# First tile's outputs from the second weight as loaded, in float32 products; the weight's split moved one step on

## The reference

```
attention:  a = softmax(causal(q k^T / 8));  local = a @ v            32 heads (4 x 8), 576 rows, 64 columns
            mem = (phi(q) @ M_prev) / (phi(q) . z_prev)
            x = g * mem + (1 - g) * local                             -> x: 2304 x 512
stage 1:    h = x @ w_in                                              512 -> 1024
            solu = h * softmax(h);  ln = (solu - mean) / sqrt(var + 1e-6) * g_ln
            y = ln @ w_out                                            1024 -> 512
stage 2:    out = (sigmoid(y @ w_gate) * (y @ w_val)) @ w_out2        512 -> 1536 -> 512
```

## Time and profile before

| | |
|---|---|
| median of 3 runs | 836.41 us (835.51 to 836.73) |
| the profiled execution | 835.18 us |
| its span | 833.4 us |
| PE busy | 814.7 us (98%) |
| DVE busy | 604.4 us (73%) |
| ACT busy | 465.4 us (56%) |
| POOL busy | 20.7 us (2%) |
| granted TensorE clock, mean | 0.998 |

### The profile page before, as it was taken

How to read it: one execution, slowest core, us unless ns; L and a number is a source line. 1 busy time by engine, 2 the same in 40 slices (tenths; PEclk the granted TensorE clock), 3 DMA queues, 4 the chain that set the end, 5 groups by cost and what they waited for, 6 DMA issues and landing times.

```text
span 833.4 us, 15447 instructions
## 1 busy us (share of the span) xinstructions
PE 814.7 (98%) x5718; PEld 688.1 (83%) x5718; DVE 604.4 (73%) x1460; ACT 465.4 (56%) x965; POOL 20.7 (2%) x35
## 2 busy tenths in 40 slices
PE   7997999999999999999999999999999999999998
PEld 4555777777777778888899999999999999999997
DVE  7988888777777775686656777787677678666654
ACT  7988666666666653463535454564444465444443
POOL 1000000000000000111000000000000000000000
PEclk9999999999999999999999999999999999999999
DMA  7362011111111000100323011122111113111002
GB/s 217 93 194 61 17 52 53 53 52 54 53 50 39 26 17 15 52 1 1 101 77 126 26 51 52 52 61 98 45 52 50 52 42 111 51 52 51 26 1 77
DMA packets 67370, 48.99 MB, mean 59 GB/s; under 512 B 9568, under 2 KB 57952, under 8 KB 67296
## 3 DMA queue, kind: packets, MB, share of 16 engines
q1 hardware_dynamic: 67152, 47.74, 19.2%
q10 hardware_dynamic: 144, 0.26, 0.1%
HBM read 43.27 MB, written 4.72 MB: 58 GB/s over the span
## 4 chain that ended last, share of the span: by engine, by line
PE 89%; DVE 5%; SPq 2%; issue 2%; ACT 1%; DMA 1%; DVEq 0%; ACTq 0%
PE tt_bk L1622 10%; PE tt_bk L1624 10%; PE tt_bk L1623 10%; PE m_bk L1467 9%; PE s_bk L1491 7%; PE o_bk L1491 5%; PE tt_bk L1390 4%; PE s_bk L1674 3%; PE s_bk L1675 3%; PE s_bk L1673 3%; PE o_bk L1398 3%; PE s_bk L1326 3%; PE m_bk L1674 2%; PE m_bk L1675 2%; PE s_bk L1467 2%; PE m_bk L1673 2%
## 5 line engine op out<-in xcount | busy, mean ns | idle before, releaser
L1622 PE MATMUL tt_bk<-xc_hi,wc_hi 128*128 128x384 f32 x476 | 160.0, 336 | 0.0
L1624 PE MATMUL tt_bk<-xc_hi,wc_lo 128*128 128x384 f32 x476 | 160.0, 336 | 0.0
L1623 PE MATMUL tt_bk<-xc_lo,wc_hi 128*128 128x384 f32 x476 | 159.8, 336 | 0.0
L598 ACT ACTIVATE p_nat<-p_nat,negmax 128x512 f32<-128x512 f32 (+2 forms) x144 | 83.0, 578 | 46.6 <-DVE negmax L931 46.6
L1166 DVE TENSOR_TENSOR wc_lo<-wc_raw,wc_hi 128x768 fp32r<-128x768 f32 x72 | 78.3, 1088 | 31.9 <-ACT wc_hi L663 31.9
L1622 PEld LDWEIGHTS tt_bk<-xc_hi,wc_hi 128*128 128x128 f32 x476 | 89.4, 188 | 6.4 <-DVE c_u L1182 0.3
L1623 PEld LDWEIGHTS tt_bk<-xc_lo,wc_hi 128*128 128x128 f32 x476 | 89.4, 188 | 6.1
L1624 PEld LDWEIGHTS tt_bk<-xc_hi,wc_lo 128*128 128x128 f32 x476 | 89.4, 188 | 0.0
L663 ACT CAST wc_hi<-wc_raw 128x768 fp32r<-128x768 f32 x72 | 64.5, 946 | 1.3 <-DVE wc_raw L1160 1.3
L605 ACT COPY pT<-tt_bk 128x512 f32<-128x512 f32 (+1 forms) x87 | 46.0, 554 | 29.2 <-PE tt_bk L1390 27.8
L1390 PE MATMUL tt_bk<-ident,p_nat 128*128 128x128 f32 x400 | 56.0, 277 | 2.6 <-DVE pT L975 1.4
(11 more groups left out here) (219 smaller groups left out, 1773.7 us busy)
## 6 DMA issues: line engine op xcount, KB each, us to landing
wc_raw<-in_moe_w_val SPq DMA_DIRECT2D x36, 256.0 KB, 3.0
wc_raw<-in_moe_w_gate SPq DMA_DIRECT2D x36, 256.0 KB, 3.4
qkT<-in_q SPq DMA_DIRECT2D x15, 288.0 KB, 2.9
v_raw<-in_v SPq DMA_DIRECT2D x16, 256.0 KB, 2.7
qkT<-in_k SPq DMA_DIRECT2D x15, 256.0 KB, 3.2
out<-o_sb SPq DMA_DIRECT2D x15, 256.0 KB, 2.2
w_raw<-in_moe_w_out SPq DMA_DIRECT2D x12, 256.0 KB, 4.7
turned<-in_k SPq DMA_DIRECT2D x32, 72.0 KB, 2.6
```

The source lines that it names most:

```text
L598: nc.scalar.activation(p_tile(g, tile), p_tile(g, tile), ACT.Exp, bias=negmax[:, n:n + 1], scale=-1.0, accum_out=den[:, n:n + 1]).then_inc ...
L1622: mm(o, hi[:, k, c, :], xc_hi[:, j, c, :], start=start and c == 0, stop=False, skip_group_check=True)
L1623: mm(o, hi[:, k, c, :], xc_lo[:, j, c, :], start=False, stop=False, skip_group_check=True)
L1624: last = mm(o, lo[:, k, c, :], xc_hi[:, j, c, :], start=False, stop=c == 1, skip_group_check=True)
```

## The change

Tile 0's outputs are no longer made of three split products. VectorE's new `first_ln` multiplies the turned rows by `g_ln` into `u_even`, and TensorE's new `first_out` multiplies that with the loaded blocks of `w_out` in float32: 8 products instead of 24. ScalarE's and VectorE's split of tile 0's rows goes. The split of `w_out`, first needed by tile 1 now, moves: on both engines blocks 0 and 1 to step 5, 2 to 4 to step 6, 5 to 7 to step 7. In step 5 fill 4 of pair 4 is copied by ScalarE instead of VectorE, ahead of `moe_exp(0)`; VectorE's copy of fill 3 moves ahead of `moe_max(0)`. In TensorE's step 6 the order of `moe_hidden`, turns and outputs is another.

```diff
     def act_fills(g):
-        return [0, 2, 5, 6] if g == HP else [0, 2, 4, 5, 6]
+        return [0, 2, 4, 5, 6]
...
-        W2_HI_MID, W2_HI_X, W2_HI_TILE, W2_HI_END = {4: (0, 1)}, {5: (2, 3, 4)}, {5: (5, 6)}, {5: (7,)}
-        W2_LO_PHI, W2_LO_TILE = {4: (0, 1)}, {5: (2, 3, 4), 6: (5, 6, 7)}
+        W2_HI_X, W2_HI_TILE, W2_HI_END = {6: (2, 3, 4), 7: (5, 6, 7)}, {5: (0,)}, {5: (1,)}
+        W2_LO_MAX, W2_LO_ROWS, W2_LO_VAR = {5: (0,), 6: (2,), 7: (5, 6)}, {6: (3,), 7: (7,)}, {5: (1,), 6: (4,)}
...
 ScalarE, step(g, t)
-                if t == 1:
-                    moe_ln(t - 1)
...
                 keep_pt(g - 1, 2)
+                if t == 0:
+                    keep_pt(g - 1, 4)
                 if t == 1:
                     feature_relu(g + 1)
                 for f in W2_HI_TILE.get(g, ()):
                     split_w2(f)
                 moe_exp(t)
-                if 4 in act_fills(g - 1):
+                if t:
                     keep_pt(g - 1, 4)
...
 VectorE
+            def first_ln():
+                dve.wait_ge(g_in, 16)
+                for n in range(2):
+                    dve.wait_ge(lnt_ready, n + 1)
+                    c = slice(512 * n, 512 * n + 512)
+                    nc.vector.tensor_tensor(u_even[:, c].rearrange("p (f k) -> p f k", f=4),
+                                            t_bk[n][:, :].rearrange("p (f k) -> p f k", f=4),
+                                            g_col[:, 4 * n:4 * n + 4].unsqueeze(2).broadcast_to([P, 4, P]),
+                                            ALU.mult).then_inc(ln_lo_ok, 1)
...
-                if t:
+                if t == 1:
+                    first_ln()
+                elif t:
                     moe_ln_low(t - 1)
...
                 if t == 0:
-                    split_w2(W2_LO_TILE[g][0])
                     unit_max(g, 6)
-                    split_w2(W2_LO_TILE[g][1])
                 keep_pt(g - 1, 1)
-                if t < 2:
-                    split_w2(W2_LO_TILE[g][2 if t == 0 else 0])
+                if t == 0:
+                    keep_pt(g - 1, 3)
+                for f in W2_LO_MAX.get(g, ()):
+                    split_w2(f)
                 moe_max(t)
-                keep_pt(g - 1, 3)
-                if t == 0:
-                    keep_pt(g - 1, 4)
-                if t == 1:
-                    split_w2(W2_LO_TILE[g][1])
-                    split_w2(W2_LO_TILE[g][2])
+                if t:
+                    keep_pt(g - 1, 3)
+                for f in W2_LO_ROWS.get(g, ()):
+                    split_w2(f)
                 moe_rows(t)
                 moe_stats(t)
                 if t == 0:
                     unit_max(g + 1, 0)
                     unit_max(g + 1, 1)
+                for f in W2_LO_VAR.get(g, ()):
+                    split_w2(f)
                 moe_var(t)
...
 TensorE
+            def first_out(f0, f1):
+                if f0 == 0:
+                    pe.wait_ge(ln_lo_ok, 2)
+                    pe.wait_ge(w2_in, 16 * FB)
+                for f in range(f0, f1):
+                    last = mm(y_bank(False), u_even[:, f * P:(f + 1) * P], w2_stage(f)[:, 0, :], start=f == 0,
+                              stop=f == FB - 1)
+                if f1 == FB:
+                    last.then_inc(y_ready, 1)
...
+                if t == 1:
+                    moe_hidden(t, 12, 24)
+                    turn_p(g - 1, 0)
+                    turn_p(g - 1, 1)
+                    pe.wait_ge(max_ok, NU * g + NU - 1)
+                    first_out(0, 2)
+                    turn_p(g - 1, 2)
+                    turn_p(g - 1, 3)
+                    first_out(2, 4)
+                    turn_p(g - 1, 4)
+                    turn_p(g - 1, 5)
+                    first_out(4, 6)
+                    turn_p(g - 1, 6)
+                    first_out(6, 8)
```

More of the change, by code:

```diff
@@ L774, in early_step @@
                     exp_tile(g, n)
-                for f in W2_HI_MID.get(g, ()):
-                    split_w2(f)
                 exp_tile(g, 6)
@@ L1033, in moe_norm @@
                                         ALU.add).then_inc(ln_ok, 1)
+            def first_ln():
[7 more added lines that the diff above has]
+                                            ALU.mult).then_inc(ln_lo_ok, 1)
             def moe_ln_low(t):
                 for n in range(2):
-                    dve.wait_ge(ln_hi_ok, 2 * t + n + 1)
+                    dve.wait_ge(ln_hi_ok, 2 * (t - 1) + n + 1)
                     c = slice(512 * n, 512 * n + 512)
@@ L1062, in early_step @@
                     split_w1(c)
-                for f in W2_LO_PHI.get(g, ()):
-                    split_w2(f)
             def step(g, t):
@@ L1565, in step @@
                     scores(g, 3)
[L1566 to L1572, removed]
+                if t != 1:
+                    m = (15, 21) if t == 0 else (18, 24)
+                    moe_hidden(t, 12, m[0])
+                    turn_p(g - 1, 0)
+                    turn_p(g - 1, 1)
+                    moe_hidden(t, m[0], m[1])
+                    turn_p(g - 1, 2)
+                    turn_p(g - 1, 3)
                 if t == 0:
                     moe_hidden(t, 21, 24)
-                if t:
+                if t > 1:
                     if g < PAIRS:
@@ L1580, in step @@
                     moe_out(t - 1, 0, 6)
-                turn_p(g - 1, 4)
-                turn_p(g - 1, 5)
-                if t:
+                if t != 1:
+                    turn_p(g - 1, 4)
+                    turn_p(g - 1, 5)
+                if t > 1:
                     moe_out(t - 1, 6, 12)
-                turn_p(g - 1, 6)
-                if t:
+                if t != 1:
+                    turn_p(g - 1, 6)
+                if t > 1:
                     moe_out(t - 1, 12, 24)
+                if t == 1:
+                    moe_hidden(t, 12, 24)
+                    turn_p(g - 1, 0)
+                    turn_p(g - 1, 1)
+                    pe.wait_ge(max_ok, NU * g + NU - 1)
+                    first_out(0, 2)
+                    turn_p(g - 1, 2)
+                    turn_p(g - 1, 3)
+                    first_out(2, 4)
+                    turn_p(g - 1, 4)
+                    turn_p(g - 1, 5)
+                    first_out(4, 6)
+                    turn_p(g - 1, 6)
+                    first_out(6, 8)
                 if t and g < PAIRS:
```

## The result

The changed kernel took 840.4 us (839.02 to 841.14, 6 runs) beside 835.79 us of the kernel before (835.46 to 836.73, 6 runs): ratio 1.005, 95% interval 1.004 to 1.006. The forecast was +3.4 us, to 839.8; measured are +4.6 and +3.7. It is slower, inside the stated range (837.0 to 841.8 us), by a little more than forecast.

What follows compares the result with a forecast made beforehand. TensorE, busy 98% of the span, was taken as the bound. `scores(6, 3)` moves from 103.89 to 107.3 us, +3.4 us carried to the end: 836.41 becomes 839.8 us, with an 8-in-10 range of 837.0 to 841.8.

Steps and rivals of the forecast that it cites:

- Step 4's splits: Step 4 to first half of step 5: ScalarE loses two splits, so work up to `turn_p(4, 4)` starts 1.22 us earlier.
- The wait of 1.44 us and what takes its place: Turns of pair 4: the wait goes, turn 6 waits for ScalarE's copy; the 2.7 us won are lost before `weighted(4)`.
- Block 0 ahead of `moe_max(0)`: Step 5: VectorE's low part waits for ScalarE's split; `moe_max(0)` 1.13 us later, TensorE idle some 3.7 us before `weighted(4)`.
- Block 1 ahead of `moe_var(0)`: VectorE's low part waits for ScalarE's split: `moe_var(0)` 3.79 us later, the turns of tile 0 +3.2 us.
- The products: Step 6, `first_out`: eight float32 products of two instructions each, 0.87 us apiece, 7.0 us for eight.
- The rival of fast products: Step 6: float32 products at the speed of a turn, 3.3 us for eight; 837.1 us, chance 0.08.
- The wait of 0.92 us for the memory part: Step 6, ahead of the turns of pair 5: the memory part is copied by 96.7, so this wait goes.
- The clock: Gap before `weighted(4)`: half speed for 3.5 us, up to 1.75 us lost but hidden; if late, 841.6 us, chance 0.09.
- Step 6: Ahead of `first_out`: TensorE waits for `max_ok` of unit 5, adding 0.2 us to the 3.2 us coming in.
- Step 7: Six splits of blocks 5 to 7 move in, unfelt on TensorE; 0.4 us at most if cover is gone.
- The rival of hidden splits: Steps 5 and 6: the splits don't hold up `moe_max(0)` or `moe_var(0)`; 1.2 us won, 835.2 us, chance 0.10.

Runs made afterwards that it cites:

- e7: The changed kernel again, unaltered, in a second comparison with the kernel before on another chip: 840.14 us, ratio 1.0039.
- e9: The kernel before, its three split products kept, with the splits of `w_out` spread elsewhere, none in step 4: 835.58 us, ratio 0.9992.
- e8: The kernel before with only the change's moves of the copies of fills 3 and 4 of pair 4: 836.15 us, ratio 0.9996.
- e1: The changed kernel with VectorE's low part of block 0 behind `moe_max(0)` instead of ahead of it: 837.87 us, ratio 1.0017.
- e4: The changed kernel with 14 products of no use on TensorE in the gap ahead of `weighted(4)`: 839.39 us, ratio 1.0044.
- e5: The kernel before with only `first_ln` and the 8 float32 products of `first_out` for tile 0; splits, copies and turns as before: 837.82 us, ratio 1.0016.
- e2: The changed kernel with VectorE's low part of block 1 moved to step 6, ahead of `moe_max(1)`: 838.96 us, ratio 1.0037.
- e3: The changed kernel with block 0's low part behind `moe_max(0)` and block 1's in step 6: 835.84 us, ratio 0.9996.
- e11: e3 with the loads of the second weight behind the load of v for pair 3: 835.4 us, ratio 0.9993.
- e10: e9 with the second weight's loads behind that of v and VectorE's block 4 ahead of `moe_max(1)`: 835.32 us, ratio 0.9990.

## Why the prediction was right, and where a size was off

*Step 4's splits.* Forecast 1.22 us; the stretch to turn 4 is 1.11 us shorter (1.31 in e7), and the wait ahead of the first hidden product is gone (67.70, no wait, against 1.36 in the earlier trace rows). Right. That this gain hangs on a load was not seen: the text named SP's queue nowhere, and the load of v behind the eight of `w_out` was the next to be late (e9).

*The wait of 1.44 us and what takes its place.* Right, and e8 shows it alone: no gain. Turn 6 did wait for ScalarE's copy (0.33 us).

*Block 0 ahead of `moe_max(0)`.* Forecast: `weighted(4)` 6.4 us behind turn 4 (82.47 - 76.09) and some 3.7 us idle. Measured 6.47 and 3.57. `moe_max(0)` starts at 80.66, which less the 1.91 us by which this profile is late is 78.75; forecast 78.65. e1 takes the wait away: 4.41.

*Block 1 ahead of `moe_var(0)`.* Forecast 3.79 us later than before; the distance from turn 4 to `moe_var` grew from 5.88 (83.19 - 77.31) to 10.87 us (88.98 - 78.11), by 4.99; less the 1.11 won up to turn 4 that is 3.88. e4 shows the wait for `ln_ok` in the open with 1.89 us, forecast 2.1.

*The products.* Forecast 0.87 us each from the weighting rows; measured 0.86, with 8.94 us for the stretch from `first_out` to `scores(6, 3)` where 9.1 were forecast. The rival of fast products is out. Alone they cost 1.26 us (e5). The wait of 0.92 us for the memory part is gone, as forecast.

*The clock: the term that was mis-sized.* The text took the fall as "hidden", at 1.75 us of lost work against 2.1 us of slack, from the 3.5 us of low clock at the start of the trace. It stayed low for about 7 us, twice as long, and the stretch from `weighted(4)` to the turns of tile 0 took 7.45 us in place of 4.59: 2.86 us. The slack took 2.0 of it, 0.9 stood out (0.65 in e7), and that part is missing in e4, which fills the gap. The place was forecast as the likely one; the length was not. In e2 it was the short one again. The section "What's actually happening" of "TensorE: Matmul & The Clock Gate" in the Trainium skill (activity releases the throttle, idleness brings it back) agrees: in e4 activity alone, of no use, kept the clock at 1.00. No run here shows what makes the low stretch long or short.

*Step 6.* The wait for `max_ok` of unit 5, forecast with 0.2 us, is absent in the changed kernel and there in e4 (0.24): TensorE came to that point about 0.8 us later than forecast and VectorE did not. So half or more of the clock's cost was given back, and that the sum came out within 0.4 us in the stretches (3.75, or 3.29 in e7, against 3.4) owes something to this: two small errors offset each other.

*Step 7.* Nothing to see: from 112 us on TensorE has one wait of 0.4 us, as before. The six splits were free.

*The rival of hidden splits.* It priced the change without the two waits at 1.2 us less than before, 835.2 us. e3 has -0.26 us in the stretches, because of the wait for v; e11, without that, has -1.06 us and 835.4 us.

The first comparison has 4.6 us where the profiles have 3.3 to 3.75 in the four stretches; the second (3.7 us) closes most of that. The rest, up to 0.9 us, is not settled; the start of the kernel, at low clock for 3.5 us in one execution and for 10 in another, scatters by as much.

## What to carry to other kernels

Before a piece of work is put in front of a short operation on the critical chain, ask what it waits for, not what it costs: two operations of 0.66 us cost about 4 us, because each waited for an operation that another engine had further down its list. A gap on TensorE may be paid a second time by the clock. What that costs depends on the slack behind it: 1.3 us or more in e1, 0.1 to 0.4 us net in the changed kernel, where TensorE had another wait to lose. A wait just removed should be followed to the next one on the same engine before it is counted as a gain. When a stage moves forward, check the loads behind the longest transfer in the queue.

## What the runs showed of the hardware

- Behind an idle stretch of 3.57 us the clock was low for about 7 us in two profiles and 3.5 us in a third; behind one of 1.90 us (e1), with 1.50 us idle some 6 us earlier, for about 3.5 us; behind one of 2.04 us (e9) for about 3.5 us; and not at all in e3 and e8, with 1.50 and 1.07 us idle. 14 products of no use inside the 3.6 us (e4) kept it at full, and there it held behind the next idle stretch of 1.89 us too.
- A float32 product on the whole array, 128x512, is two instructions with starts 0.43 us apart and a recorded duration of 0.592 us; three float32r products of the same size take 0.69 us (3 x 0.23), so one float32 product costs a quarter more than the three it replaces, and saves the splits.
- A load of v issued right behind the eight loads of `w_out` (256 KB each) landed 4.9 to 7.3 us after its issue (ten profiles); issued ahead of them it landed after 2.6 to 2.7 us (e10, e11).
- VectorE's product with a factor broadcast along the columns, out of PSUM, takes as long as the subtraction that it replaced (two in 1.29 us, two in 1.28 before).
- The start scatters. The clock falls at 11 to 14 us in every profile. It stays low for about 3.5 us in nine of them, for 7 us in that of e5, and for 10 us in that of e10 and the first of the changed kernel, whose TensorE reached step 5 1.9 us later than before's. Of 70 further runs of the kernel before, 21 had a mean granted clock of 0.997 or 0.998 and took 834.96 to 836.02 us (median 835.4), 49 had 0.993 to 0.996 and took 836.05 to 837.28 us (median 836.6). That these 1.2 us are the start's is not shown for runs without a profile, but they are a third of the effect studied, and more than the gain of the best version.
